# A fused linear-attention and MLP kernel on Trainium2: key decays taken from the decay mask, the first head's loads put first in the queue, and its products inside chunks put ahead of the next head's scores

## The reference, cut to what matters

```
for b in range(nb):
    intra = (q_b @ k_b.T) * Dmask                 # Dmask[i, j] = lam ** (i - j) for i >= j, else 0
    out_b = intra @ v_b + (q_b * lam ** (pos + 1)) @ kv_state
    kv_state = lam ** block * kv_state + (k_b * lam ** (block - 1 - pos)).T @ v_b
```

## Time and profile before

| | |
|---|---|
| median of 3 runs | 575.38 us (574.7 to 575.71) |
| profiled execution | 575.11 us |
| its span | 573.3 us |
| TensorE busy | 563.9 us (98%) |
| VectorE, ScalarE, GpSimd busy | 360.9, 253.3, 242.8 us |

### The profile page before, as it was taken

One profiled execution on the slowest core, in us unless ns is written; L12 is line 12 of the kernel. 1 busy time (PEld: TensorE's weight loads), 2 busy tenths in 40 slices (PEclk: granted clock), 3 DMA queues, 4 the chain that ended last, 5 costly groups with the idle time before them and its releaser, 6 DMA issues.

```text
span 573.3 us, 9532 instructions
## 1 busy us (share of the span) xinstructions
PE 563.9 (98%) x3602; PEld 501.8 (88%) x3602; DVE 360.9 (63%) x634; ACT 253.3 (44%) x510; POOL 242.8 (42%) x241
## 2 busy tenths in 40 slices
PE   7999999999999999999999999999999999999997
PEld 6899887988989898899969888998898898899996
DVE  5676868676643796276978963769864543444333
ACT  2565334555643454334553534354554334444430
POOL 3341236366643453304667542047563332323311
PEclk9999999999999999999999999999999999999999
DMA  8980111422222120211112212211222212221142
GB/s 308 371 324 3 73 38 40 120 81 83 83 84 66 64 71 22 74 56 33 60 55 74 75 21 72 57 54 39 75 73 75 71 58 74 74 67 57 42 147 111
DMA packets 24157, 49.11 MB, mean 86 GB/s; under 512 B 2472, under 2 KB 3632, under 8 KB 24112
## 3 DMA queue, kind: packets, MB, share of 16 engines
q1 hardware_dynamic: 23520, 46.70, 24.5%
q0 software_dynamic: 448, 1.71, 1.0%
q10 hardware_dynamic: 144, 0.10, 0.1%
HBM read 45.35 MB, written 3.15 MB: 85 GB/s over the span
## 4 chain that ended last, share of the span: by engine, by line
PE 81%; DVE 14%; issue 2%; ACT 1%; DMA 1%; SPq 0%; DVEq 0%; ACTq 0%
PE banks L1100 13%; PE banks L1101 13%; PE banks L1099 13%; PE banks L1365 10%; PE banks L1367 10%; PE banks L1368 10%; DVE al L705 2%; PE banks L1178 2%; PE banks L1124 2%; PE banks L1187 2%; DVE u L875 2%; PE banks L1160 2%; DVE h0l L778 1%; PE banks L1203 1%; DVE snap L992 1%
## 5 line engine op out<-in xcount | busy, mean ns | idle before, releaser
L338 POOL TENSOR_TENSOR w2l<-raw,w2h 128x512 fp32r<-128x512 f32 x56 | 74.7, 1334 | 155.8 <-ACT w2h L453 155.8
L1365 PE MATMUL banks<-th,al 128*128 128x384 f32 x392 | 132.2, 337 | 1.8 <-DVE sums L705 1.3
L1367 PE MATMUL banks<-tl,ah 128*128 128x384 f32 x392 | 132.4, 338 | 0.0
L1368 PE MATMUL banks<-th,ah 128*128 128x384 f32 x392 | 132.2, 337 | 0.0
L453 ACT ACTIVATE snap<-banks 128x384 f32<-128x384 f32 x84 | 41.2, 490 | 129.9 <-PE banks L1368 129.6
L705 DVE TENSOR_TENSOR al<-raw,ah 128x512 fp32r<-128x512 f32 (+1 forms) x112 | 86.6, 794 | 5.4 <-ACT ah L453 4.0
L992 DVE TENSOR_TENSOR snap<-banks,snap 128x384 f32<-128x384 f32 x84 | 46.4, 552 | 65.8 <-PE banks L1368 65.2
L1365 PEld LDWEIGHTS banks<-th,al 128*128 128x128 f32 x392 | 73.7, 188 | 10.7 <-issue 3.5
L1367 PEld LDWEIGHTS banks<-tl,ah 128*128 128x128 f32 x392 | 73.6, 188 | 5.9
L1368 PEld LDWEIGHTS banks<-th,ah 128*128 128x128 f32 x392 | 73.7, 188 | 0.0
L338 POOL TENSOR_TENSOR raw<-raw 128x256 f32<-128x256 f32 x84 | 69.4, 842 | 2.2
(11 more groups left out here) (172 smaller groups left out, 893.1 us busy)
## 6 DMA issues: line engine op xcount, KB each, us to landing
raw<-w1b_dram SPq DMA_DIRECT2D x16, 512.0 KB, 3.5
raw<-w2b_dram SPq DMA_DIRECT2D x32, 256.0 KB, 3.2
raw<-w1a_dram SPq DMA_DIRECT2D x12, 512.0 KB, 3.5
raw<-w2a_dram SPq DMA_DIRECT2D x24, 256.0 KB, 3.4
kTs<-kT_dram SPq DMA_DIRECT2D x8, 384.0 KB, 6.3
qTs<-qT_dram SPq DMA_DIRECT2D x8, 384.0 KB, 7.3
kns<-kn_dram SPq DMA_DIRECT2D x8, 384.0 KB, 7.8
vns<-vn_dram SPq DMA_DIRECT2D x8, 384.0 KB, 5.5
```

The costliest lines, as they stand in the source:

```text
L338: return nc.gpsimd.tensor_tensor(o, i0, i1, ALU.subtract)
L1365: mm(o[:, 0:HALF], al[:, a, cols], th[b][:, t, k, :], start=start and k == 0, stop=False, skip_group_check=True)
L1367: mm(o[:, 0:HALF], ah[:, a, cols], tl[b][:, t, k, :], start=False, stop=False, skip_group_check=True)
L1368: last = mm(o[:, 0:HALF], ah[:, a, cols], th[b][:, t, k, :], start=False, stop=(k == 1), skip_group_check=True)
```

## The change

1. `lrev`, `ex`, their loads, the power instruction and their semaphores are removed. `decay_k(h)` takes its factor from the last column of the mask, `dmask[:, h % 3, 127]`, which holds the same powers, and so waits for `decay_rows(h)`. That needs the rows one step earlier: `decay_rows(h+2)` in step h, from h = 0. From head 3 on it also waits until the keys that read the slot before are done. Spacers keep the addresses of the other buffers.
2. `lamb` is loaded from ScalarE's queue, ahead of `ident`, so SyncE's list begins with the first head's loads; for that head `vns` stands ahead of `kns`.
3. On TensorE the products inside chunks of head 0 and then `state_products(0)` stand ahead of `scores(1)`. `keep_warm(4)` is gone and `WARM` is 3 rather than 4. From head 1 on the order is the same.

```diff
-WARM = 4
+WARM = 3
...
-            sp.dma_start(lamb[:, :], lam.partition_broadcast(L)).then_inc(s_lam, 16)
-            sp.dma_start(ex[:, :, :], expo).then_inc(s_ex, 16)
             for h in range(H):
...
-                sp.dma_start(kns[:, i, :, :], kn[h].rearrange("p (c n) -> p c n", c=NC)).then_inc(s_k[i], 16)
+                if h:
+                    sp.dma_start(kns[:, i, :, :], kn[h].rearrange("p (c n) -> p c n", c=NC)).then_inc(s_k[i], 16)
                 if p >= 0:
                     sp.wait_ge(att_done, p + 1)
                 sp.dma_start(vns[:, i, :, :], vn[h].rearrange("p (c n) -> p c n", c=NC)).then_inc(s_v[i], 16)
+                if h == 0:
+                    sp.dma_start(kns[:, i, :, :], kn[h].rearrange("p (c n) -> p c n", c=NC)).then_inc(s_k[i], 16)
...
-            pool.wait_ge(s_lam, 16)
-            pool.wait_ge(s_ex, 16)
...
-            nc.gpsimd.tensor_tensor(lrev[:, :], lamb[:, :], ex[:, 0, :], ALU.pow).then_inc(lrev_ready, 1)
             nc.gpsimd.memset(mhalf[:, :], -0.5)
...
             def decay_k(h):
                 act.wait_ge(s_k[h % NI], loaded(h) // 2)
+                act.wait_ge(dmask_ready, h + 1)
                 if h >= 2:
                     act.wait_ge(kv_done, h - 1)
-                copy(kdec[:, h % 2, :, :], kns[:, h % NI, :, :], scale=lrev[:, h:h + 1]).then_inc(kdec_ready, 1)
-
+                copy(kdec[:, h % 2, :, :], kns[:, h % NI, :, :], scale=dmask[:, h % 3, L - 1:L]).then_inc(kdec_ready, 1)
+
+            act.dma_start(lamb[:, :], lam.partition_broadcast(L)).then_inc(s_lam, 16)
             act.dma_start(ident[:, :], idpad).then_inc(s_id, 16)
...
-            act.wait_ge(lrev_ready, 1)
             decay_k(0)
...
                 if h >= 3:
                     dve.wait_ge(mask_done, 2 * (h - 2))
+                    dve.wait_ge(kdec_ready, h - 2)
...
-                if h and h + 1 < H:
-                    decay_rows(h + 1)
+                if h + 2 < H:
+                    decay_rows(h + 2)
                 states(h)
...
             scores(0)
-            pe.wait_ge(s_id, 16)
-            state_products(0)
-            keep_warm(4)
...
+            def within_chunks(h):
+                pe.wait_ge(s_v[h % NI], loaded(h) // 2)
                 for c in range(NC):
                     if c % NA == 0:
                         pe.wait_ge(mask_done, 2 * h + c // NA + 1)
...
+            within_chunks(0)
+            state_products(0)
+            pe.wait_ge(s_id, 16)
+            for h in range(H):
+                if h + 1 < H:
+                    scores(h + 1)
+                else:
+                    pe.wait_ge(mask_done, 2 * H)
+                    mix_half(0, 0, range(4), 0)
+                if h:
+                    turn(h - 1)
+                    within_chunks(h)
                 if h + 1 < H:
                     state_products(h + 1)
```

More of the change, by code:

```diff
@@ L73, in build @@
         lamb = sb(ctx, "lamb", [L, H])
-        ex = sb(ctx, "ex", [L, 3, H])
+        sb(ctx, "spacer3", [L, 24])
         raw = sb(ctx, "raw", [L, 6, 512])
@@ L77, in build @@
         ident = sb(ctx, "ident", [L, 64 + L])
-        lrev = sb(ctx, "lrev", [L, H])
-        sb(ctx, "spacer2", [L, 64])
+        sb(ctx, "spacer2", [L, 72])
         mv = sb(ctx, "mv", [L, B, NA, 2, 2])
@@ L176, in build @@
         warm_ready, warm_done = sem("warm_up_zeros_ready"), sem("warm_up_done")
-        s_lam, s_ex, s_id = sem("lam_loaded"), sem("expo_loaded"), sem("ident_loaded")
+        s_lam, s_id = sem("lam_loaded"), sem("ident_loaded")
         s_tokw = sem("tokmix_weights_loaded")
@@ L184, in build @@
         s_erow, erow_zero = sem("edge_rows_loaded"), sem("edge_rows_zeroed")
-        lrev_ready, row_ready, dmask_ready = sem("lrev_ready"), sem("lam_row_ready"), sem("decay_mask_ready")
+        row_ready, dmask_ready = sem("lam_row_ready"), sem("decay_mask_ready")
         chain, ends_ready = sem("dve_chain"), sem("row_ends_ready")
@@ L1127, in scores @@
                     last.then_inc(sc_done, 1)
-            def keep_warm(n):
-                for _ in range(n):
-                    mm(bank[7][:, 0:L], ident[:, 64:64 + L], ident[:, 64:64 + L], start=True, stop=True)
             pe.wait_ge(warm_ready, 1)
```

## The result

| | before | changed |
|---|---|---|
| median | 575.32 us (574.57 to 576.65, 18 runs) | 577.0 us (575.45 to 579.6, 18 runs) |
| ratio, 95% interval | | 1.0028 (1.0018 to 1.0038) |
| profiled execution, span | 575.11, 573.3 us | 579.6, 577.8 us |

The changed kernel is 1.7 us slower, where 1.5 us less was forecast. The profiled execution happens to be the slowest of its 18, 2.6 us above the median, so its sizes are read with care: they show where time can be lost, not how much of it is lost on average. The distance between lowest and highest time has grown, from 2.1 to 4.2 us.

What follows compares the result with a forecast made beforehand. TensorE, holding 81% of the chain, was taken to bound the kernel. At `scores(2)`, 0.95 us of slack plus 0.6 from the queue gave 1.5 won: 575.38 - 1.5 = 573.9 us, range 573.0 to 575.2.

Steps and rivals of the forecast that it cites:

- The queue term: Start of the kernel: every large load up to head 2 comes 0.6 us earlier by moving `lamb` off SyncE's queue.
- The bounds of 0.3 to 0.91: Lower and upper limit, in us, on how much earlier the large loads up to head 2 come.
- The cover of VectorE: VectorE's idle 2.02 us before the mask at 7.50: a later `ident` costs only beyond it.
- `ident` landing later than 6 us: Sign in the changed profile that would upset the first step, the start of head 0.
- some 0.8 us: Length of `decay_rows(2)` on VectorE, from 8.72, ahead of `states(0)` and before `kv_done` at 10.15.
- The slack of `scores(2)`: At `scores(2)`: 0.95 us between its queries' load and their reader (14.64 to 15.58), used up by the moved products.
- From head 1 on each step has the same instructions, so I count nothing there: Steps from head 1 on: no gain or loss counted.
- The later load: Rival: a later load, such as head 5's queries, stops TensorE; 574.2 to 575.4 us; chance 0.15 together with a gainless queue.
- The clock: Rivals: fewer zero products leave TensorE at half rate from `scores(0)`; 574.5 us if short (0.18), 578.8 if long (0.07).
- the short slow clock: Rival: only `scores(0)` runs at half rate, 0.85 us won by `scores(2)`, 574.5 us; chance 0.18.
- The long one: Rival: all TensorE pieces of the first two heads at half rate, `scores(2)` 3.4 us later, 578.8 us; chance 0.07.

Runs made afterwards that it cites:

- e1: Changed kernel with `lamb` back as the first load on SyncE: 576.34 us, ratio 1.0016.
- e4: Changed kernel with `lamb` back as the first load on SyncE and four zero products instead of three: 575.9 us, ratio 1.0009.
- e8: e4 with TensorE's order of the kernel before and its four identity products: 575.46 us, ratio 0.9993.
- f1: e4 with the second token-mixing weights load moved from head 4 to head 7: 575.99 us, ratio 1.0013.
- f4: e4 with both token-mixing weights loads moved from head 4, the first to head 6, the second to head 7: 574.56 us, ratio 0.999.
- g4: e4 with 16 more waits on a long-set semaphore ahead of `scores(0)`: 575.52 us, ratio 1.0006.
- h1: f4 with TensorE's order of the kernel before and its four identity products: 574.44 us, ratio 0.999.
- h2: The program of f4 measured again, on the same chip as h1: 576.1 us, ratio 1.0006.
- g2: Kernel before with both token-mixing weights loads moved to heads 6 and 7: 574.99 us, ratio 0.9993.
- e2: Changed kernel with four zero products instead of three: 576.76 us, ratio 1.0022.
- e3: Changed kernel with four zero products, TensorE's order of the kernel before and its four identity products: 575.22 us, ratio 1.0.
- e6: e4 with four narrow zero products ahead of `scores(0)`: 576.16 us, ratio 1.0009.
- g1: Changed kernel with both token-mixing weights loads moved to heads 6 and 7: 576.63 us, ratio 1.0025.
- e5: Changed kernel with five narrow zero products ahead of `scores(0)`: 577.26 us, ratio 1.0026.
- f3: Changed kernel with the second token-mixing weights load moved from head 4 to head 7: 576.34 us, ratio 1.0022.
- g3: f4 with `lamb` and `ident` both first on SyncE's queue: 576.39 us, ratio 1.0027.
- f2: Kernel before with the second token-mixing weights load moved from head 4 to head 7: 575.53 us, ratio 1.0005.
- e7: Kernel before without its four identity products, `keep_warm(4)`: 575.62 us, ratio 1.0004.

## Why the prediction was wrong

- **The queue term failed, in sign.** The step is "I take 0.6 us for every large load up to head 2". The first large load was issued 0.91 us earlier, but `scores(0)` started 0.57 us later, while `lamb` and `ident` shared the engines with the keys and the rate fell to 106 GB/s. The bounds of 0.3 to 0.91 excluded a loss without a row for it, though the text itself said that `ident` had those microseconds nearly to itself. Even with the mended queue the term isn't there: the first large load is issued at 1.17, 0.48 us ahead of the kernel before, and `scores(0)` starts at 6.41 to 7.00 (e1, e4, e8, f1, f4, g4, h1, h2), against 6.42 to 6.55 in the four profiles with the early list of before. The rule that the prediction cited from the Trainium skill, page "Trainium Kernel Development and Optimization", section Key Constraints, that queues of different engines share 16 engines and interleave, pointed the right way and was only used to lower the gain.
- **The cover of VectorE ran out.** "Without that cover each microsecond that `ident` is late beyond 2.02 us would cost one": its transfer took 3.0 us longer, it landed at 7.17, and the mask's row starts at 7.19. The prediction had named this sign itself ("`ident` landing later than 6 us"). It goes away with the mended queue (4.16 in e1). One thing more comes with it: the rows, now late, meet GpSimd's products. The last scan ahead of the mask took 1.15 or 1.16 us in all six profiles with the mixed queue and 0.40 in the kernel before, and `decay_rows(2)`, put at "some 0.8 us", took 1.7 (0.73 in e1, where no product of GpSimd's runs then).
- **The slack of `scores(2)` was there, but not for certain.** With the mended queue and the new order it starts at 14.33 to 14.71 in e1, e4, g4 and h2, against 15.31 before by the same reading: 0.6 to 1.0 us, where 0.95 was named. But f1 and f4, whose list up to there is that of e4 and h2, start it at 15.58 and 15.27, behind late queries; and the kernel before's own early list gave 14.88 in g2. So the slack is collected in some executions only.
- **"From head 1 on each step has the same instructions, so I count nothing there" failed.** The same list is not the same time. By the experiments this is the largest step: the new order was to win 0.95 us and cost 1.5 with the mixed queue (e2, e3). With the mended queue it cost 1.7 with late weights (h2, h1; 0.9 by the ratios) and 0.4 with the weights where they were (e4, e8, not side by side; 0.9 by the ratios), neither clear of noise by itself. The profiles show the loss as TensorE standing still at fixed counts of its records. In the new order these pieces are 1.3 to 3.7 us in eight profiles (changed, e1, e2, e4, e6, f1, g1, h2) and 0 to 0.95 in five (e5, f3, f4, g3, g4). In the old order they are 0 to 0.7 in six (before, e3, e8, f2, g2, h1) and 1.8 in one (e7). Nor is a microsecond won on the way to the steady work one of the whole: h2 leads h1 by 0.9 us at `scores(2)` and trails it by 2.7 at the last turn. That TensorE waits for its own instructions there is the reading argued above.
- **The later load**, "1.2 us of margin; if they come at least 0.6 earlier, 1.8 are there". It was right to ask: in e5 and e8 head 5's queries stop TensorE. In the changed kernel they don't; there TensorE comes to `scores(5)` late itself.
- **The clock.** `scores(0)` took 2.84 us in the changed kernel, the weight loads' mark of the lower level as in the earlier trace rows, under a granted clock of 1.00. f3 shows the same; e1 and g1 have three zero products too, and 1.54 us; the ten further profiles with four zero products and no narrow ones have 1.54. So the short slow clock happens in some executions, and in the changed kernel it cost nearly nothing, since the mask waited for VectorE's rows anyway (9.46 in e2, 9.53 here). The long one is not in the changed kernel's profile (it is in e5's, where the products inside chunks and `scores(1)` are long too). Four of its 18 executions have a mean granted clock of 0.994, but at 576.33 to 577.75 us they lie around the median, so the clock doesn't explain the loss.

Where the loss comes from, by differences of medians: 0.2 from the missing zero product (changed to e2, not clear of noise), 1.5 from the new order with the mixed queue (e2 to e3, clear of it), and nothing from the mixed queue with the old order (e3 is at 1.0). The queue's 0.7 to 0.9 appear only in the new order, so the parts don't add up singly.

What stays open is why the blocks come late more often in the new order. A full stage is part of it at most: late weights help the new order once (f4), not a second time (h2, the same program), and not with the mixed queue (g1). In h1 and e8 the packet behind the block that starts near 22 us comes 0.4 us after it, in e4, h2, f4 and the kernel before after 3.0 to 4.5; what makes it early or late isn't known. A shift of the list alone did not do it either (e7, g4). An old order with the new one's boundaries was not tried. The new order's best execution, 573.46, is 0.5 us below the old one's, 573.96: the gain is there and is mostly not collected.

The best kernel here is h1, 0.9 us (0.15%) below the kernel before, less than the 0.2% that can be told from nothing.

## What to carry to other kernels

A load that is needed first should not get company: before a small load is moved to a second queue, ask what it does to the big ones and they to it, and let the lower bound be a loss. Where TensorE runs without a pause and the loads are near the transfer engines' rate, an earlier start is not yet a gain; look for "issue" pieces at equal distances in the engine's records, and at the spread of the runs, before the new order is believed. One profiled execution of such a kernel can be the luckiest or the unluckiest: set the two orders against each other on one chip, with everything else equal, and don't take a profile that shows the forecast time for a proof of the forecast's course.

## What the hardware showed that I had not expected

- With two small loads in ScalarE's queue beside the large ones, all transfers came to 106 to 109 GB/s for two microseconds (225 and 369 before), and `ident`'s 96 KB took 6.0 us in place of 3.0.
- TensorE's pauses of 0.1 to 2.0 us at counts of 221, 347, 472, 597 and 722 records, in different places of the program, each ended 1.2 to 1.6 us behind the end of an instruction packet of 16 KB. Mostly such a packet is seen 3 to 5 us after a block begins.
- SyncE's issue of one load took 1.44 and 1.82 us in e5 and e8, with its neighbours at 0.33 to 0.47.
- A 128x128 scan that VectorE began while GpSimd multiplied two large arrays ended 0.3 us behind the end of that product and took 0.82 to 3.0 us in place of 0.40 to 0.43; the power instruction on 128x8 (4.09 to 5.74 in the kernel before) held up no scan.
- The lower clock level showed in weight loads and in `scores(0)` (2.84 for 1.54 us) while the granted clock in the rows said 1.00 throughout.
